# Top-k attention with two MLPs on one core: the mask moves from two GpSimd subtractions to one accumulating DMA

## The reference

```python
scores = scale * np.matmul(q, k.transpose(0, 1, 3, 2))     # scale = 1/8
kth = np.partition(scores, -top_k, axis=-1)[..., -top_k:-top_k + 1]   # top_k = 32
scores = np.where(scores >= kth, scores, -1000000000.0)
scores = scores - np.max(scores, axis=-1, keepdims=True)
attn = np.exp(scores)
attn = attn / (np.sum(attn, axis=-1, keepdims=True) + 1e-09)
x = np.matmul(attn, v)            # (B*S, 512) after a transpose
g = np.maximum(x @ w_in, 0.0) ** 2
x = g @ w_out                     # then the routed MLP on x
```

## Time and profile before

| | |
|---|---|
| median of 3 runs | 923.28 us |
| span of the profiled execution | 920.5 us |
| PE busy | 885.1 us, 96% |
| DVE busy | 819.2 us, 89% |
| ACT busy | 658.5 us, 72% |
| POOL busy | 656.6 us, 71% |
| DMA | 175.40 MB, mean 191 GB/s |
| mean granted PE clock | 0.985 |

### The profile page before, as it was taken

How to read it: one execution, slowest core, us unless ns; L and a number is a source line. 1 busy time by engine, 2 the same in 40 slices (tenths; PEclk the granted TensorE clock), 3 DMA queues, 4 the chain that set the end, 5 groups by cost and what they waited for, 6 DMA issues and landing times.

```text
span 920.5 us, 21085 instructions
## 1 busy us (share of the span) xinstructions
PE 885.1 (96%) x6684; PEld 719.2 (78%) x6684; DVE 819.2 (89%) x2584; ACT 658.5 (72%) x1297; POOL 656.6 (71%) x884
## 2 busy tenths in 40 slices
PE   4799899999999999999999999999999999999997
PEld 2677687888888788888788887888878886788886
DVE  6999999999999999999999999999991064888887
ACT  3777787777777778777777777877775322788886
POOL 2999998878887787787888778778787452444432
PEclk7799999999999999999999999999999999999999
DMA  9962533566344658866535455433533675764990
GB/s 332 364 242 95 173 125 124 166 203 193 120 166 142 212 181 280 239 188 229 170 130 169 138 186 171 169 125 125 189 125 114 242 243 208 273 226 154 335 334 23
DMA packets 69750, 175.40 MB, mean 191 GB/s; under 512 B 21298, under 2 KB 26418, under 8 KB 65280
## 3 DMA queue, kind: packets, MB, share of 16 engines
q1 hardware_dynamic: 67568, 168.77, 54.2%
q0 software_dynamic: 1840, 5.06, 1.7%
q10 hardware_dynamic: 224, 0.15, 0.1%
HBM read 154.19 MB, written 21.27 MB: 191 GB/s over the span
## 4 chain that ended last, share of the span: by engine, by line
PE 84%; DVE 11%; POOL 2%; issue 1%; ACT 1%; DMA 0%; DVEq 0%; SPq 0%; POOLq 0%
PE psum L1352 8%; PE psum L1417 7%; PE psum L1418 7%; PE psum L1419 7%; PE psum L1377 7%; PE psum L1434 7%; PE psum L1435 7%; PE psum L1396 7%; PE psum L1436 7%; DVE top L1052 3%; DVE upper L1057 3%; PE psum L1650 2%; PE psum L1619 2%; PE psum L1624 2%; PE psum L1655 2%; PE psum L1658 2%
## 5 line engine op out<-in xcount | busy, mean ns | idle before, releaser
L1052 DVE MAX8 top<-upper 128x8 f32<-128x288 f32 x576 | 238.8, 446 | 0.0
L629 POOL TENSOR_TENSOR s_sb<-s_sb,below 128x576 f32<-128x576 f32 x144 | 203.3, 1434 | 1.5 <-ACT below L801 1.5
L1057 DVE MATCH_REPLACE8 upper<-top,upper 128x288 f32<-128x288 f32 x432 | 187.6, 441 | 0.0
L1417 PE MATMUL psum<-x_high,w_in_high 128*128 128x256 f32 x576 | 168.3, 292 | 1.6 <-POOL x_low L635 1.1
L1418 PE MATMUL psum<-x_low,w_in_high 128*128 128x256 f32 x576 | 161.8, 281 | 0.0
L1419 PE MATMUL psum<-x_high,w_in_low 128*128 128x256 f32 x576 | 161.2, 280 | 0.0
L792 ACT ACTIVATE s_sb<-psum 128x576 f32<-128x576 f32 x144 | 93.8, 651 | 93.7 <-PE psum L1352 84.2
L644 POOL TENSOR_TENSOR square<-relu 128x256 f32<-128x256 f32 x144 | 89.7, 623 | 81.7 <-ACT relu L834 80.9
L649 POOL TENSOR_TENSOR g_low<-square,g_high 128x256 fp32r<-128x256 f32 x144 | 108.4, 753 | 30.3 <-POOL square L644 23.2
L1352 PE MATMUL psum<-k_sb,q_sb 64*128 64x288 f32 x512 | 100.1, 469 | 21.7 <-DVE lower L1043 19.1
L801 ACT ACTIVATE below<-s_sb,steep_kth 128x576 f32<-128x576 f32 x144 | 110.8, 770 | 9.2 <-POOL neg_max L617 8.4
(11 more groups left out here) (213 smaller groups left out, 1848.0 us busy)
## 6 DMA issues: line engine op xcount, KB each, us to landing
w_ring<-w_split SPq DMA_DIRECT2D x144, 512.0 KB, 4.5
weights<-w SPq DMA_DIRECT2D x32, 1024.0 KB, 7.1
v_sb<-v_main SPq DMA_DIRECT2D x48, 256.0 KB, 2.5
w_split<-w_ring SPq DMA_DIRECT2D x16, 512.0 KB, 4.3
k_sb<-kT SPq DMA_DIRECT2D x32, 144.0 KB, 4.5
k_sb<-kT SPq DMA_DIRECT2D x32, 128.0 KB, 4.3
weights<-w_out SPq DMA_DIRECT2D x1, 4096.0 KB, 13.5
weights<-w_in SPq DMA_DIRECT2D x1, 4096.0 KB, 21.1
```

The source lines that it names most:

```text
L629: nc.gpsimd.tensor_tensor(s_sb[:, s % SBUFS, n, 0:S], s_sb[:, s % SBUFS, n, 0:S], below[:, n, :], ALU.subtract).then_inc(masked, 1)
L1052: v.max(top[:, s % 2, n, 8 * r:8 * r + 8], upper[:, s % 2, n, :]).then_inc(upper_step, 1)
L1057: v.match_replace(upper[:, s % 2, n, :], top[:, s % 2, n, 8 * r:8 * r + 8], upper[:, s % 2, n, :], LOWEST).then_inc(upper_step, 1)
L1417: t_.matmul(dst, wh, x_high[:, j % 2, k, :], start=k == 0, stop=False)
```

## The change

The scores are kept negated in `s_sb`, so that masking is an addition of `below`. One DMA for each step, issued by POOL with `accum_op=ALU.add`, adds both tiles of `below` to both tiles of `s_sb`; the two subtractions of `mask` are gone. The issue stands in POOL's order between `normalise(t-2, 0)` and `normalise(t-2, 1)`, and waits for both `find_below` of its step. The semaphore `masked` now counts 16 for each step, and both `exponentiate` of a step wait for all of it. The scale factors follow: the copies scale by -1/8, the bounds by 1/8, the exponential takes scale -1, and `find_upper` and `find_lower` compare unscaled scores, with the operands from `s_sb` and from PSUM exchanged.

```diff
@@ set_bounds
-                nc.gpsimd.tensor_scalar(steep_kth[:, s % 2, :], kth[:, s % 2, :], STEEP, 1.0,
+                nc.gpsimd.tensor_scalar(steep_kth[:, s % 2, :], kth[:, s % 2, :], STEEP, SCALE,
                                         ALU.mult, ALU.mult).then_inc(bias_set, 1)
-                nc.gpsimd.tensor_scalar(neg_max[:, s % 2, :], top[:, s % 2, :, 0], -1.0, 1.0,
+                nc.gpsimd.tensor_scalar(neg_max[:, s % 2, :], top[:, s % 2, :, 0], -1.0, SCALE,
@@ mask
-            def mask(s, n):
-
-                pool.wait_ge(below_set, 2 * s + n + 1)
-                nc.gpsimd.tensor_tensor(s_sb[:, s % SBUFS, n, 0:S], s_sb[:, s % SBUFS, n, 0:S], below[:, n, :],
-                                        ALU.subtract).then_inc(masked, 1)
+            def mask(s):
+
+
+                pool.wait_ge(below_set, 2 * s + 2)
+                pool.dma_start(s_sb[:, s % SBUFS, :, :].rearrange("p n s -> p (n s)"), below[:, :, :].rearrange("p n s -> p (n s)"),
+                               accum_op=ALU.add).then_inc(masked, 16)
@@ POOL's loop
                     normalise(t - 2, 0)
+                if 0 <= t - 1 < NS:
+                    mask(t - 1)
+                if 0 <= t - 2 < NS:
                     normalise(t - 2, 1)
                 if 0 <= t - 3 < NS:
                     split_x(t - 3)
-                if 0 <= t - 1 < NS:
-                    mask(t - 1, 0)
-                    mask(t - 1, 1)
@@ copy_scores, find_below, exponentiate
-                                     scale=SCALE).then_inc(scores_copied, 1)
+                                     scale=-SCALE).then_inc(scores_copied, 1)
...
-                wait(act, masked, 2 * (s - 1) + n + 1)
+                wait(act, masked, 16 * s)
...
-                                     scale=-STEEP).then_inc(below_set, 1)
+                                     scale=STEEP).then_inc(below_set, 1)
...
-                act.wait_ge(masked, 2 * s + n + 1)
+                act.wait_ge(masked, 16 * (s + 1))
...
-                nc.scalar.activation(tile, tile, ACT.Exp, bias=neg_max[:, s % 2, n:n + 1],
+                nc.scalar.activation(tile, tile, ACT.Exp, bias=neg_max[:, s % 2, n:n + 1], scale=-1.0,
@@ find_upper (find_lower alike, with ALU.min)
-                v.scalar_tensor_tensor(out=upper[:, s % 2, :, :], in0=score_banks(s, 1), scalar=SCALE,
-                                       in1=s_sb[:, s % SBUFS, :, 0:HALF], op0=ALU.mult, op1=ALU.max).then_inc(upper_set, 1)
+                v.scalar_tensor_tensor(out=upper[:, s % 2, :, :], in0=s_sb[:, s % SBUFS, :, 0:HALF], scalar=-1.0 / SCALE,
+                                       in1=score_banks(s, 1), op0=ALU.mult, op1=ALU.max).then_inc(upper_set, 1)
```

More of the change, by code:

```diff
@@ L67, in build @@
     SCALE = float(HD) ** -0.5
+    assert SCALE == 0.125
     QT_FULL = S // P
@@ L1035, in find_upper @@
                 wait(dve, upper_step, 14 * (s - 1))
-                v.scalar_tensor_tensor(out=upper[:, s % 2, :, :], in0=score_banks(s, 1), scalar=SCALE,
-                                       in1=s_sb[:, s % SBUFS, :, 0:HALF], op0=ALU.mult, op1=ALU.max).then_inc(upper_set, 1)
+                v.scalar_tensor_tensor(out=upper[:, s % 2, :, :], in0=s_sb[:, s % SBUFS, :, 0:HALF], scalar=-1.0 / SCALE,
+                                       in1=score_banks(s, 1), op0=ALU.mult, op1=ALU.max).then_inc(upper_set, 1)
             def find_lower(s):
                 wait(dve, lower_step, 6 * (s - 1))
-                v.scalar_tensor_tensor(out=lower[:, s % 2, :, :], in0=score_banks(s, 1), scalar=SCALE,
-                                       in1=s_sb[:, s % SBUFS, :, 0:HALF], op0=ALU.mult, op1=ALU.min).then_inc(lower_set, 1)
+                v.scalar_tensor_tensor(out=lower[:, s % 2, :, :], in0=s_sb[:, s % SBUFS, :, 0:HALF], scalar=-1.0 / SCALE,
+                                       in1=score_banks(s, 1), op0=ALU.mult, op1=ALU.min).then_inc(lower_set, 1)
             def upper_max(s, r, n):
```

## The result

The changed kernel takes **1318.8 us** (median of 4 runs, 1316.2 to 1320.6) against 923.2 us: 1.429 times, 95% interval 1.427 to 1.431. The forecast was 1240 us in a range of 1070 to 1500.

What follows compares the result with a forecast made beforehand. PE and DVE pace the 9.53 us step; the loop through ACT and POOL grows to 6.65 + 7.3 = 13.95 us (13.05 in the first 9 intervals), adding 316.8 us to the 920.5 us span: 1240 us, range 1070 to 1500.

Steps and rivals of the forecast that it cites:

- the spent cover: Loop through ACT and POOL: 8.1 us against the pacers' 9.33 us; the change spends this cover of about 1.2 us.
- The length from X to the next B: On ACT, from the start of a step's first exponentiate to the end of the next second find_below: 6.65 us.
- Edits at nothing: Negated scores, other scale factors and exchanged operands of find_upper and find_lower were costed at nothing.
- G: Time that POOL is held by issuing the mask's DMA, taken as 1.15 us from the scatters.
- The landing: Term two: exponentiate waits for the mask's DMA, 7.3 us from the end of the second find_below to its landing.
- term one: Place of the issue: the second normalise waits behind it on POOL, delaying PE, rectify and exponentiate; loop 11.0 us by this path.
- The short landing: Rival, 14%: the DMA lands within 4.4 us, so the place of the issue decides; 11.04 us a step, 1035 us.
- The PE clock: Rival, 6%: PE's standstill before the second half of transpose_probs keeps its clock low, so PE paces again; 1386 us.
- The slow accumulation: Rival, 12%: landing takes 11.9 us or more, from dearer bytes, shared engines or a slow adder; 1566 us.
- Faster: Rival, 2%: transfer and its wait at exponentiate wholly hidden, DVE's and PE's pace stays; 909 us.
- no change: Rival, 2%: the DMA is not what holds, its wait is met early or ordered otherwise; 923 us.
- Intervals of 14 us: Sign in the changed trace: find_kth on DVE starts about every 14 us, 13 in the first ten.

Runs made afterwards that it cites:

- sign_only: The changed kernel without the DMA: POOL masks with two additions at their old place, negated scores, scale factors and exchanged operands kept; 922.9 us, ratio 0.9999.
- place_only: The changed kernel without the DMA: POOL masks with two additions at the DMA's place, ahead of the second normalise; 1384.7 us, ratio 1.501.
- place_clock18: place_only with 18 matmuls of the identity put into PE's wait for the second normalise; 1258.6 us, ratio 1.364.
- dma_late: The changed kernel with the accumulating DMA issued behind both normalise and split_x, the old place of the mask; 1205.9 us, ratio 1.305.

## Why the prediction was right, and where it was not

**What bounds the kernel, and the spent cover: right.** Busy shares said that POOL was not the bound, and the loop through ACT and POOL had 1.2 us of cover. The length from X to the next B was put at 6.65 us; in the 35 steps with a late landing it is 6.51 us. This term carried the forecast, and holds within 0.2 us.

**Edits at nothing: right**, by sign_only.

**G, the hold on POOL: 1.15 us forecast, 0.90 measured.** The nearest row for a POOL-issued DMA, the scatters', was near enough. That the second `normalise` ends at B + 2.0 where the forecast had B + 1.94 is partly luck: the issue starts 0.30 us after B and not 0.05, and this `normalise` takes 1.06 us where 0.74 was put. In place_only it takes 0.75 us, so it is longer only behind the issue of a DMA; why is open.

**The landing: right in the mean, for a reason that the sum didn't have.** L was 7.3 us, from 4.5 us for 256 KB and the doubled bytes. Undisturbed it is 5.1 us from B and 4.8 us from the issue, with the add; the base of 4.5 us, taken from gathers and scatters, was too much, since a whole 576 KB lands in 3.0 us from the issue as a copy. In the 35 late steps it is 9.24 us from B. The mean, (35 x 9.24 + 27 x 5.44) / 62 = 7.6 us, is within 0.3 of the forecast, but by luck, for two errors cancel: the base was too high, and the disturbance by `w_ring` was no term of the sum, only a word in the slow rival. The doubling itself held, 366 against 179 ns a packet. The Trainium skill ("Collectives: The Full Stack", section "The bandwidth ceiling: the fold count and why AG ≠ RS ≠ AR") gives the two source reads as the cause, and both numbers agree with its factor of 2; that it is the reads, no run here shows. The Trainium skill's page "DMA: Bandwidth & Descriptors", section "Anatomy of one DMA — SWDGE (gpsimd) path", would give 3.4 us as an estimate for these bytes: near the 3.0 us of the undisturbed copy, well under the 4.8 us of the undisturbed addition.

**The step that failed: term one.** The prediction saw that the second `normalise` would move behind the issue and that PE's work stands behind it, but followed it only as far as `rectify` and X (3.24 + G). It didn't follow the same wait around the loop that closes through PE: from `normalise` through all of PE's work for the step and ACT's copies to the next B, 10.4 us at the full clock in most steps and 10.6 in the mean. With the 2.0 us where `normalise` ends that is 12.4 to 12.6 us, not 11.0, and with the clock 14.6 us. The part that it did follow, 2.45 us from the end of `normalise` to X, holds at the full clock (place_clock18: 6.15 - 3.59 = 2.56 us) and not at the lower one (place_only, the same order: 7.72 - 3.57 = 4.15 us). So X comes mostly 6.3 us after B in the even steps of the changed kernel, where this path gave 4.4. The two paths compete in each step, and a step lasts as long as the longer one. The numbers add up: the 35 late steps were 15.78 - 13.95 = 1.83 us longer than forecast, +64 us; the 27 early ones would have lasted 5.44 + 6.4 = 11.84 us by the landing, -57 us; the loop through PE lifts these to 14.59 us, +74 us. The sum is +81 us, and 1318.4 less the forecast span of 1237.3 is 81 us. The rest, the first nine steps (+2 us) and what lies outside the 71 intervals (7 us where 11 were put), nearly cancels.

**The rivals.** The short landing (14%) named the place as what decides below 4.4 us, at 11.04 us a step: the landing isn't that short, and the price was wrong for the reason above. The PE clock (6%) was taken to be hidden in PE's idle time unless it kept PE full. That is wrong: the clock costs at least 36 us in the changed kernel, and 126 us where only the place differs, with PE far from full. The sentence that the lower clock fits in the 4 us that PE idles was wrong because PE idles ahead of the work that the low clock then slows, and that work is in the loop. The slow accumulation (12%), at 1566 us, has its mechanism in half of the steps: sharing with the `w_ring` loads. Faster and no change were rightly given 2% each.

**The signs.** Intervals of 14 us: 15.3, and 13.3 in the first nine, where 13 was put. PE's wait of 3 us ahead of the second transposes: 2.8 to 2.9. A landing after 7.2 us: 6.1 in the median, from 4.8 to 11.2. DVE idle before the reciprocal: in each step. ACT's wait for the DMA: in 35 of the odd steps and 6 of the even ones.

In all, of 396 us: 283 us are what the DMA costs with the old order (dma_late), some 72 of these for the addition and 80 for the `w_ring` loads ahead of it, each taken away alone; 113 us more are the place. These shares hold in this order only, since place_only alone loses 462 us. No version with the DMA came under 1086 us, and none that masked fully under 1122 us. A further delay of the exponential by one step, with a fifth buffer for the scores, might hide the landing, but PE and DVE would still pace at 9.3 us or more, so it can at best be even with before; it was not tried.

## What to carry to other kernels

To relieve an engine that isn't the bound gains nothing by itself: what replaces its work must have a shorter way from the last input to the first user, not less busy time. When an instruction is moved up in an in-order engine, follow the wait that it brings through every engine that stands behind it and around each loop until it closes, and compare the loops; here the first user was not on the longest way. A wait on PE of about 3 us in each step, as here, also has to be priced with the clock that it loses for the work behind it.

## What the runs showed of the hardware that was not expected

- A DMA with an addition took 366 ns for a packet of 4608 bytes where a copy took 179 ns, and its issue held POOL for 0.90 in place of 0.59 us.
- A DMA issued by POOL waited behind SP's large loads: its first packet started 1.47 us after the issue when SP's queue was quiet and mostly 3.5 to 5 us after it when 1 MB of `w_ring` had just been issued; 27 of the 56 steps of the table started more than 3 us late.
- With PE waits of 2.8 to 2.9 us, one in each step of 14 to 16 us, and shorter ones beside them, the granted clock was at 1.2 GHz for 4 to 6 us of each step; 18 matmuls of no use in a wait of 4.3 us kept it at 2.4 GHz and made the kernel 126 us faster.
